# Unread products on PE in two routings, and four splits moved behind the second

## The reference

```
x = attention(q, k, v)               # 2304 tokens x 512
# first mixture (8 experts, 512 -> 1024 -> 512)
e   = argmax(x @ w_gate);  g = softmax(x @ w_gate)[e];  o = sigmoid(x @ w_output_gate)[e]
x   = g * o * (relu(x @ w1[e]) @ w2[e])
# second mixture: the same without o, and an expert takes its first `capacity` tokens only
out = g * (relu(x @ w1[e]) @ w2[e])  # 0 for a token over the capacity
```

## Time and profile before

| | us |
|---|---|
| median of 3 runs | 753.04 (751.76 to 753.70) |
| profiled execution | 754.11 |
| its span, first to last instruction | 752.4 |
| PE busy (matmul) | 642.0 (85%) |
| DVE busy | 356.8 (47%) |
| POOL busy | 419.8 (56%) |
| ACT busy | 180.3 (24%) |
| mean granted clock of PE | 0.929 |

### The profile page before, as it was taken

The page is one execution under the profiler, slowest core; times in us unless marked ns, Lnnn a source line. Parts: engine busy times, 40 slices in busy tenths (PEclk is TensorE's granted clock), DMA queues, the critical chain, the costliest instruction groups (busy, mean ns, idle before and its releaser), DMA issues.

```text
span 752.4 us, 15054 instructions
## 1 busy us (share of the span) xinstructions
PE 642.0 (85%) x4310; PEld 529.1 (70%) x4311; DVE 356.8 (47%) x652; ACT 180.3 (24%) x223; POOL 419.8 (56%) x351
## 2 busy tenths in 40 slices
PE   4898855999999999999987534999999999998653
PEld 3787844788887888877876423788888878886542
DVE  3887745454354354354334084545454364433240
ACT  2577631002420112422322200022023200243200
POOL 1046442256685657779778342116657763579760
PEclk9999985999999999999998655999999999999796
DMA  9999993043444425445554313114325532355500
GB/s 198 233 297 283 271 337 125 29 140 137 157 156 152 154 79 174 175 154 186 178 176 155 110 37 104 44 34 153 126 87 177 182 126 84 112 174 195 191 32 21
DMA packets 79690, 111.64 MB, mean 148 GB/s; under 512 B 28249, under 2 KB 46681, under 8 KB 79664
## 3 DMA queue, kind: packets, MB, share of 16 engines
q1 hardware_dynamic: 67616, 86.00, 37.0%
q0 software_dynamic: 8000, 25.17, 9.9%
q10 hardware_dynamic: 4048, 0.12, 0.3%
HBM read 92.48 MB, written 20.00 MB: 150 GB/s over the span
## 4 chain that ended last, share of the span: by engine, by line
PE 50%; POOL 14%; issue 12%; DVE 10%; POOLq 5%; DMA 5%; ACT 1%; ACTq 1%; DVEq 0%; SPq 0%
PE b L998 12%; PE b L999 12%; POOL wl L423 12%; PE b L1000 12%; PE b L925 2%; PE b L1020 2%; PE b L993 2%; PE b L903 2%; DVE owner L773 1%; DVE kT L665 1%; POOLq L423 1%; PE b L1045 1%; DVE xrow L676 1%; DMA x<-y,sidx 1%; PE b L913 1%
## 5 line engine op out<-in xcount | busy, mean ns | idle before, releaser
L423 POOL TENSOR_TENSOR wl<-ring,wh (+1 forms) x128 | 302.0, 2386 | 43.0 <-issue 21.3
L607 ACT CAST wh<-ring 128x1024 f32 (+1 forms) x112 | 112.8, 1047 | 479.2 <-PE b L1000 387.3
L998 PE MATMUL b<-wh,xTh 128*128 x320 | 135.0, 422 | 5.7 <-DVE xTl L814 3.7
L998 PE MATMUL b<-wh,hTh 128*128 x320 | 132.5, 414 | 7.5 <-DVE hTl L827 7.5
L842 DVE TENSOR_SCALAR y<-b,gates 128x512 f32<-128x512 f32 x40 | 30.0, 751 | 227.0 <-PE b L1000 103.2
L999 PE MATMUL b<-wh,xTl 128*128 x320 | 129.0, 403 | 0.0
L999 PE MATMUL b<-wh,hTl 128*128 x320 | 128.9, 403 | 0.0
L1000 PE MATMUL b<-wl,xTh 128*128 x320 | 128.0, 400 | 0.0
L1000 PE MATMUL b<-wl,hTh 128*128 x320 | 127.9, 400 | 0.0
L804 DVE TENSOR_SCALAR h<-b 128x512 f32<-128x512 f32 x80 | 54.8, 689 | 78.3 <-PE b L1000 78.1
L998 PEld LDWEIGHTS b<-wh,hTh 128*128 128x128 f32 x320 | 61.8, 193 | 21.3 <-issue 7.7
(11 more groups left out here) (142 smaller groups left out, 663.1 us busy)
## 6 DMA issues: line engine op xcount, KB each, us to landing
ring<-in_moe_w SPq DMA_DIRECT2D x128, 512.0 KB, 3.2
vin<-in_v SPq DMA_DIRECT2D x72, 64.0 KB, 4.9
x<-xrow POOLq DMA_DIRECT2D x18, 256.0 KB, 6.1
out<-zeros SPq DMA_DIRECT2D x18, 256.0 KB, 3.8
qin<-in_q SPq DMA_DIRECT2D x6, 512.0 KB, 7.5
kin<-in_k SPq DMA_DIRECT2D x6, 512.0 KB, 6.9
qin<-in_q SPq DMA_DIRECT2D x2, 384.0 KB, 5.6
kin<-in_k SPq DMA_DIRECT2D x2, 384.0 KB, 5.9
```

The source lines that it names most:

```text
L423: nc.gpsimd.tensor_tensor(low, src, high.bitcast(F32), ALU.subtract).then_inc(wl_here, 1)
L607: nc.scalar.copy(dst, ring[:, i % RING]).then_inc(wh_here, 1)
L998: nc.tensor.matmul(dst, high, weights(wh, *wt), start=start, stop=False)
```

## The change

PE gets products whose result nobody reads: `unread(n)` multiplies two constant tiles (`below`, 128x128, and 512 columns of `iota_b`, bf16) into `b23`, n times, without a wait. In each routing such a block stands in front of every wait of PE: 6 (first) or 30 (second) before `onehot_ready`, 14 or 17 before the slot products, 4 before the gate products, 8 before `routed`, and 5 between the transposes of tile 0 and its first product. And the four splits that POOL made between gather 0 and gather 1 of the second mixture are taken out there; `done` says 76 in place of 80, so that POOL's loop makes them.

```diff
@@ POOL, between the gathers
                 gather_first(0)
                 if m == 1:
-                    for i in range((E + 1) * PX + PW, (E + 2) * PX):
-                        low_parts(i, i % RING)
                     pool.wait_ge(s_zero, 16 * NT)
                 gather_first(1)
@@ DVE, in the routing
-                done = FIRST if m == 0 else (E + 2) * PX
+                done = FIRST if m == 0 else (E + 1) * PX + PW
@@ PE
+            def unread(n):
+
+                for _ in range(n):
+                    nc.tensor.matmul(b23[:, 0:BANK], below[:, :], iota_b[:, 0:BANK // 8, 0:8],
+                                     start=True, stop=True)
+
             for m in range(2):
 
+                unread((6, 30)[m])
                 pe.wait_ge(onehot_ready, m + 1)
...
+                unread((14, 17)[m])
                 for k in range(2):
                     pe.wait_ge(at_ready, 2 * m + k + 1)
...
                 last.then_inc(slot_done, 1)
+                unread(4)
                 for k in range(2):
                     pe.wait_ge(gates_at, 2 * m + k + 1)
...
                 last.then_inc(gates_done, 1)
+                unread(8)
                 pe.wait_ge(routed, m + 1)
...
                         rows_T(0)
+                        unread(5)
                         first, before = expert_of(0)
```

## The result

The changed kernel took 744.32 us in the median of 4 runs (742.29 to 745.90), the kernel before 753.37 in the same series (751.76 to 755.91): 9.05 us faster, ratio 0.9875 with a 95% interval of 0.9839 to 0.9912. The time lies in the predicted range (735 to 744.5), but only 0.2 us under its upper end, and one of the four runs lies above it; the forecast was 739.2.

A forecast was written before the change was run, and what follows sets the result against it. The two routings were taken as the bound: PE waits at low clock on short DVE instructions, `owner` stalled behind splits. Stall 9.8 plus clock 4.0 gave 13.8 us, from the median 753.04 to 739.2 us; range 735 to 744.5.

The forecast's parts named there:

- The stall: Second routing: with the splits gone, `owner` falls from 10.02 to 0.18 us and tile 0's transposes come 9.81 us earlier.
- The moved splits: Second mixture, step 1, ahead of scatter 0 and gather 4: the four splits cost 0, bounds 0 and 9.24 us.
- The unread products' price: PE in both routings: 0.23 us each at full clock, 0.43 at the lower level; at full clock a cost of 0.
- What the clock gives back: Both routings and tile 0's products: a faster PE clock saves 2.0 us a routing, 4.0 for both; at most 3.4 each.
- the case without the fall: Both routings: the clock stays full from the first blocks through tile 0's products, saving 3.4 us a routing at most.
- What arrived at the end: Whole span: nothing after the routings depends on absolute time, so both gains, 13.8 us, should arrive at the end.
- rival (b): Both routings: the stall goes but the clock falls and late blocks take what tile 0 gains; 743.2 us, chance 0.21.
- Rival (a): Both routings: the clock holds at full speed throughout, 16.6 us gained; 736.4 us, chance 0.22.
- (c): Second mixture, step 1: the moved splits delay scatter 0, `y` and PE, so 9.24 us come back; 748.4 us, chance 0.07.
- (d): Both routings: unread products never raise the clock and their overruns add 12.8 us; 756.0 us, slower, chance 0.04.

The follow-up runs named there:

- e1_splits_only: Kernel before with the four splits moved out of the second routing as in the change, no unread products; 744.09 us, ratio 0.9828.
- e3: Kernel before with two of the four splits moved out of the second routing and two left there, no unread products; 752.04 us in one run.
- e7: Kernel before with the four splits kept between gather 0 and gather 1 but made to wait for `routed`, no unread products; 748.86 us in one run.
- e4_fill: Changed kernel with 19 and 22 instead of 14 and 17 unread products before the slot products, one more between their halves; 744.35 us, ratio 0.9839.
- e2: Changed kernel with the four splits put back between the gathers and `done` at 80, unread products kept; 755.43 us, ratio 0.9991.
- e5: Changed kernel without the unread blocks of four and of eight; 743.31 us in one run.
- e6: e4_fill with the eight divided: four between the halves of the gate products, four behind them; 743.58 us, ratio 0.9823; run again, 740.88 us, ratio 0.9796.
- e8: e6 with its unread products in the second routing only; 745.17 us, ratio 0.9847.

## Why the prediction was right, and where not

*The stall: right.* 9.81 predicted, 9.85 measured where nothing else was changed (`xg 2` of e1_splits_only against the earlier trace rows). That it was the splits is shown by e3 and e7. `routed` released the transposes in e1_splits_only, not the gather, which I had last by 0.03 us; at such a distance either may be (it was the gather in e7).

*The moved splits: right, at 0.* They ran in step 1 between gather 3 and scatter 0; `y` of tile 1 was 0.35 us late (0.5 computed), and nothing behind it.

*The unread products' price: nearly.* One took 0.43 at the lower level as assumed and 0.25 at full clock (22 in 5.50 us, e4_fill's second routing) instead of 0.23. The 215.7 ns that the prediction quotes from the Trainium skill was not met, and at 215.7 ns the eight would not quite have fitted either (1.73 us in 1.70). At full clock the blocks fit except the eight, which put `xg` 0.2 us later.

*What the clock gives back: the term that was mis-sized.* Forecast 2.0 us a routing, on the choice that the fall between the blocks comes in half the cases. It came in all four routings of the two profiles of the changed kernel, and in the four of e2 and e5, which have the same blocks ahead of the slot products: eight of eight, each time during the second nine slot products or before the gate products.

Against the kernels with no unread product in that routing (first 27.34 in the mean of seven profiles, second 27.43 in the mean of two with the splits moved) the changed kernel's 26.88 and 25.96, and 27.50 and 26.61, save 0.9 and 0.4 us, 1.3 in place of 4.0. That is near what the working gave for the fall, 0.5 to 0.9 a routing, and it is small beside the spread of its base: without unread products the first routing took 26.8 to 27.8, in step with when the clock rose, 4.0 to 6.2 us behind tile 0's first product. So the mechanism of the fall was foreseen, and the even chance given to it was the error; an average of two cases was forecast where each execution takes one of them. The late blocks were priced rightly for that case: tile 0's transposes 2.3 us late, and 1.5 to 2.1 measured.

For the case without the fall the price was too high. With the gaps filled and the long rows of short products broken (e6) the clock saves 2.7 and 2.1 us a routing against the 3.4 worked out. One reason is that the slot products save nothing (below). Another is that without the stall the clock rose 4.0 to 4.2 us into tile 0's products in the second routing (e1), where I had taken the 5.7 of the first for both, so fewer of them ran low.

*What arrived at the end: not foreseen.* The prediction has both gains arrive whole. In the profiles the two routings save 11.1 us and the span 8.2, since attention and the end of the second mixture, which the forecast holds equal, were 3.2 us longer.

So of the cases rival (b) is what happened: the fall in both routings, with the late blocks taking most of what tile 0 gains. That its 743.2 lies so near the measured 744.3 is in part luck, since the stages that nobody changed spread by more than the whole term of the clock; so is it that the time is inside the range, by 0.2 us. Rival (a) exists, but not in this kernel. Rivals (c) and (d) did not come; unread products do raise the clock.

## What to carry to other kernels

The DVE instruction of 0.2 us that took 10 was waiting for something that isn't a semaphore. In such a case look at what POOL does from its start to its end, and move that work behind the last DVE instruction of the chain, not only behind the blocked one. Look where PE is left with short products alone. With the blocks of the change the clock fell there in eight of eight routings; with the gap filled and blocks between the halves (e6, and e8's second routing) it held in five of five. A block that stands behind such a fall costs 1.7 times its length (0.43 against 0.25 us a product): fill the gaps before it, or leave the later blocks out. Where a stage that wasn't touched spreads by more than the effect, compare stages inside the profiles, and run the two versions on one chip.

## What the runs showed of the hardware

Short bf16 products did not go faster at the full clock: nine of 56 columns took 1.15 us with the clock full (117.54 in the profile after) and 1.16 at the lower level, and eighteen of 84 columns 3.02 to 3.04 in both (e4_fill). I had counted 0.3 us for the second nine.

`owner` began 0.7 us before the first split's start by the profile and was held all the same, though in the first routing it ran in 0.18 us beside a gather; what POOL holds in that time is not shown by any run.

The Trainium skill ("SBUF — State Buffer", section "Who interferes with whom") has a GpSimd instruction and a DVE instruction in a 2-port form exclude each other for the whole instruction, the one that issues first holding the ports. e3 agrees that DVE is fully blocked, and adds that a row of splits is not broken between two. On the order it doesn't fit as it stands: by the recorded starts `owner` came first and was the one held. That `owner` takes a 2-port form is not shown. Whether the DVE instructions behind `owner`, with two SBUF inputs, would have been held too was not tried.
